# Fourteen attention pair steps reordered on five engines: conversions later, scores before transposes

## The chip, the core and the metric

The kernel runs on one core of a Trainium2 chip. The metric is device time in microseconds (us). The kernel before took 1053.33 us, the median of three runs (1053.15 to 1053.75). The program is written by hand for each engine: TensorE (PE), VectorE (DVE), ScalarE (ACT), GpSimd (POOL), and the queue of transfers on SyncE (SP). Each engine runs its instructions strictly in the order written and waits on semaphores.

## The reference

```
scores = (q @ k.T) / sqrt(64)          # 4 batches, 8 heads, 768 positions
keep   = (key < 4) | (0 <= query - key < 128)
a = softmax(where(keep, scores, -1e9));  x = (a @ v) as [3072, 512]
h = x @ w_in;  x = (h - tanh(h)) @ w_out                     # 512 -> 2048 -> 512
logits = x @ w_gate + modality_bias[modality_id]
e = argmax(logits); out = softmax(logits)[e] * (relu(x @ w1[e]) @ w2[e])   # 8 experts
```

The results must hold float32 accuracy, so operands are scaled by a power of two and split into a high and a low float16 part.

## The kernel before, in words

Attention goes by **pairs**: 128 queries of two heads. A **group** g is one head pair over 384 queries, so it has three pairs, r = 3g, 3g+1, 3g+2. The first 14 pairs (`ALONE = 14`) run before the first dense layer starts; each is a **step** r of `alone`. From pair 14 on, pairs are threaded between the matmuls of the dense layers (`window`), which fill TensorE. The first dense matmul (`mlp_in`, line 805) waits for the low part of x of group 3, which pair 11 completes; it stands behind all that PE has in the 14 steps.

What a pair needs, by function and line:

- `score_pair`: PE computes scores (L607) into one PSUM tile pair, `s_ps`. It may start only when the exponentials (L635) of the pair before have read that tile. DVE masks (L621, L625, L627) and takes the row maxima (L629). ACT takes the exponentials and row sums (L635).
- `normalise`: DVE inverts the row sums (L645, L646), ACT writes the normed rows (L652). In a step with r = 3g the normed rows also wait until DVE has copied the sink columns of the group before (`gather_sinks`, L664).
- `transpose_probs`: PE transposes (L679), ACT copies the high part (L684), DVE takes the low part (L688), POOL writes the masked copies into `pt` (L694, and L697 unless r = 3g).
- `transpose_sinks`, once a group: PE (L713), ACT (L718), DVE (L722).
- `weigh_values` (PE, L760, L762) and `split_x` (ACT L782, DVE L785).

Beside the pairs stand preparations, placed by a **half step** number i (step r holds i = 2r and 2r+1). `conversions` turns group g of q and k into halves: two maxima on DVE (L406), five small scale operations and two multiplications on POOL (L417 to L421, L432), the high halves on ACT (`conv`, L449, waits for the multiplication), the low halves on POOL (L453). `prepare_alone` does the same for v (maxima L503 on DVE, multiplication L518 on POOL, high half L533 on ACT, low half L536 on POOL), the sinks' rows of v (L542, L550, L559), and both weight matrices (L296 and L311 on PE, L358 on ACT, L361 on DVE, L365 and L367 on POOL).

A row like `ACT q_hi` that waits therefore also holds back the exponentials of the next pair, since they stand behind it on ACT.

Of the kernel before, what the change touches and what calls it, by code (L numbers as in the profile page):

```python
# [125 lines left out]
def front(nc, dram, shared, attention):  # L126

    with ExitStack() as ctx:
# [76 lines left out]
        q = {n: sem("f_" + n) for n in names}  # L205
# [338 lines left out]
        def sink_halves(E, eng, b):  # L544
            s = b % 2
            if E == "act":
                eng.wait_ge(q["vs_mult"], b + 1)
                if b >= 2:
                    eng.wait_ge(q["pv_done"], pv_count(2 * PPC * (b - 1) - 1))
                eng.activation(vs_all[s][:], vs_raw[:], ACT.Copy).then_inc(q["vs_hi_done"], 1)  # L550
            if E == "pool":
                if b == 0:
                    eng.wait_ge(q["conv_lo"], 8)
                if b:
                    eng.wait_ge(q["qk_mult"], 2 * (2 * HP * b + 1))
                    eng.wait_ge(q["parted"], parts(max(r for at, r in scored.items() if at <= SLOTS * (2 * b - 2) + 22)))
                eng.wait_ge(q["vs_hi_done"], b + 1)
                low = vs_all[s][STRIP:2 * STRIP, :]
                eng.tensor_tensor(low, vs_raw[STRIP:2 * STRIP, :], low, ALU.subtract).then_inc(q["vs_lo_done"], 1)  # L559
                eng.wait_ge(q["vs_lo_done"], b + 1)  # L560
# [18 lines left out]
        def parts(r):  # L579

            return sum(1 if is_first(i) else 2 for i in range(r + 1))

        def pv_count(r):

            return sum(not is_first(i) for i in range(r + 1))
# [601 lines left out]
        def conversions(E, eng, i):  # L1187

            for g in range(1, HP * NC):
                early = {1: (None, 0, 1, 2), 2: (4, 5, 6, 7), 3: (8, 9, 10, 11), 4: (13, 14, 15, 16), 5: (19, 20, 21, 22)}  # L1190
                q_top, k_top, q_split, k_split = early.get(g, (6 * g - 11, 6 * g - 9, 6 * g - 7, 6 * g - 6))
                tops, splits = (q_top, k_top, k_top), (q_split, k_split)
                at = divmod(g, HP)
                for part in range(2):
                    if i == tops[part]:
                        qk_top_of(E, eng, *at, part)
                if i == tops[2]:
                    qk_scales(E, eng, *at)
                    qk_multiply(E, eng, *at)
                for part in range(2):  # L1200
                    if i == splits[part]:
                        conv(E, eng, *at, part)

        def prepare_alone(E, eng, i):

            for blk in {0: (0,), 1: (1, 2), 2: (3,), 3: (4, 5)}.get(i, ()):
                v_tops(E, eng, 0, blk)
            if i == 0 and E == "pool":
                late_constants(E, eng)
            if i == (3 if E == "dve" else 4) and E in ("dve", "pe"):  # L1210
                spread(E, eng, 0)
            if i == (4 if E == "dve" else 5):
                v_scales(E, eng, 0)
                for blk in range(TPC):
                    v_multiply(E, eng, 0, blk)
            if i == 8:
                for blk in range(TPC):
                    v_split(E, eng, 0, blk)
            if i == 9:
                sink_multiply(E, eng, 0)  # L1220
            if i == 11:
                sink_halves(E, eng, 0)
            if i in (18, 20, 22):
                v_multiply(E, eng, 0, i // 2 - 6)
            if i in (19, 21, 23):
                v_split(E, eng, 0, (i - 1) // 2 - 6)
            if i in (5, 6, 7, 8):
                weight_gram(E, eng, 0, i - 5)
            if i == 10:
                weight_diagonal(E, eng, 0)  # L1230
            if i == (11 if E == "pe" else 12):
                weight_product(E, eng, 0)
            w_in_at = (13, 15, 17, 19, 21, 23, 25)
            at = i - 1 if E == "dve" else i
            if at in w_in_at:
                weight_split(E, eng, 0, w_in_at.index(at))
            if i in (12, 14, 16, 18):
                weight_gram(E, eng, 1, (i - 12) // 2)
            if i == 19:
                weight_diagonal(E, eng, 1)  # L1240
            if i == (20 if E == "pe" else 21):
                weight_product(E, eng, 1)
            if i == 22:
                batch_scales(E, eng, 0)
            if i in (23, 26):
                weight_split(E, eng, 1, (23, 26).index(i))
            if i == 26:
                if E == "dve":
                    late_constants(E, eng)
# [49 lines left out]
        def stage(work_on, E, eng, r, *more):  # L1299
            if r is not None and 0 <= r < PAIRS:  # L1300
                work_on(E, eng, r, *more)

        def alone(E, eng):

            weighed = {5: (1,), 7: (2,), 8: (4, 5)}
            if E in ("pe", "dve"):
                score_pair(E, eng, 0)
            conversions(E, eng, 0)
            for r in range(ALONE):
                if E == "pe":  # L1310
                    stage(transpose_probs, E, eng, r - 1)
                    if r + 1 < ALONE:
                        score_pair(E, eng, r + 1)
                    for of in weighed.get(r, (r - 2,) if r > 8 else ()):
                        stage(weigh_values, E, eng, of)
                if E == "act":
                    score_pair(E, eng, r)
                    stage(transpose_probs, E, eng, r - 1)
                    normalise(E, eng, r)
                if E == "dve":  # L1320
                    normalise(E, eng, r)
                    if r + 1 < ALONE:
                        score_pair(E, eng, r + 1)
                    stage(gather_sinks, E, eng, r - 1)
                    stage(transpose_probs, E, eng, r - 1)
                if E == "pool":
                    stage(transpose_probs, E, eng, r - 1)
                for i in (2 * r, 2 * r + 1):
                    if i:
                        conversions(E, eng, i)  # L1330
                    if i == 2 * r + (E in ("act", "dve")):
                        stage(transpose_sinks, E, eng, r - 1)
                    if i == 2 * r:
                        for of in weighed.get(r, (r - 2,) if r > 8 else ()):
                            stage(split_x, E, eng, of)
                    prepare_alone(E, eng, i)

        scored = {2 * (r - ALONE): r for r in range(ALONE)}

# [921 lines left out]
```

## Time and profile before

| | value |
|---|---|
| median of three runs | 1053.33 us |
| profiled execution, its own time | 1051.26 us |
| its span, first to last instruction | 1049.7 us |
| first scores to first dense matmul (14 pair steps) | 8.34 to 88.81 us |
| mean granted TensorE clock, whole span | 0.974 of full speed |
| PE busy in the span | 963.0 us, 92% |
| DVE, ACT, POOL busy | 59%, 51%, 43% |

The profiled execution is the one whose rows are shown; its span leaves 1.6 us of its time uncovered. A timeline row gives start, duration, engine, line and operation; in brackets stands how long the engine had stood idle before the row and which instruction ended that wait. Durations of neighbouring rows overlap a little, because an engine takes its next instruction before the last results have landed.

### The profile page before, as it was taken

How to read it: one execution, taken by the hardware profiler on the slowest of the kernel's cores; microseconds unless marked ns; L12 is line 12 of the kernel's file. 1: busy time of each engine (PE TensorE's matmuls, PEld its weight loads, DVE VectorE, ACT ScalarE, POOL GpSimd, SP SyncE). 2: the span in 40 equal slices, each digit the busy share in tenths (PEclk: the TensorE clock that was granted, in tenths of full speed). 3: DMA queues.
4: the chain of work that ended last, by engine and by line, in shares of the span. 5: the costliest groups of instructions: out<-in, count | busy, mean ns of one | idle time of the engine just before them, and what ended most of it. 6: DMA issues, size and time to landing. Idle time of an engine off the chain costs nothing.

```text
span 1049.7 us, 23285 instructions
## 1 busy us (share of the span) xinstructions
PE 963.0 (92%) x7646; PEld 605.3 (58%) x7646; DVE 617.0 (59%) x1573; ACT 532.2 (51%) x1329; POOL 454.1 (43%) x760
## 2 busy tenths in 40 slices
PE   3447988999999999999999999999899999899996
PEld 2333544565555565565556556555577777677773
DVE  7454876668666757776756765547584334732321
ACT  4445776656656665655665665446422223522221
POOL 5755887735535643545653631210132322222322
PEclk9776999999999999999999999999999999999998
DMA  9503121314411323322122221050215112111111
GB/s 348 190 18 108 47 62 39 101 43 129 102 47 42 90 65 108 86 67 59 42 75 58 73 60 29 2 201 21 28 35 202 51 50 55 31 50 40 50 50 39
DMA packets 50293, 78.51 MB, mean 75 GB/s; under 512 B 14688, under 2 KB 35680, under 8 KB 48672
## 3 DMA queue, kind: packets, MB, share of 16 engines
q1 hardware_dynamic: 41312, 64.01, 20.5%
q0 software_dynamic: 5728, 13.43, 4.2%
q8 instruction: 43, 0.70, 0.3%
q10 hardware_dynamic: 3168, 0.02, 0.2%
q14 instruction: 42, 0.34, 0.1%
HBM read 45.35 MB, written 14.12 MB: 57 GB/s over the span
## 4 chain that ended last, share of the span: by engine, by line
PE 69%; DVE 9%; POOL 8%; issue 6%; ACT 4%; DVEq 1%; DMA 1%; SPq 1%; ACTq 0%; POOLq 0%
PE acc L861 18%; PE h_ps L805 17%; PE h_ps L1986 5%; PE s_ps L1935 5%; PE pt_ps L1935 5%; PE acc L1986 5%; PE x_out L760 3%; PE s_ps L612 3%; PE s_ps L912 2%; PE pt_ps L679 1%; POOL pt L694 1%; POOL v_lo L536 1%; POOL v_raw L518 1%; POOL qk_raw L432 1%; PE x_out L1912 1%
## 5 line engine op out<-in xcount | busy, mean ns | idle before, releaser
L861 PE MATMUL acc<-w_out_all,g_hi 128*128 128x512 f16 x768 | 228.6, 379 | 0.0
L805 PE MATMUL h_ps<-xt_hi,w_in_all 128*128 128x384 f16 x960 | 197.2, 329 | 5.7 <-DVE g_raw L826 4.5
L861 PE MATMUL acc<-w_out_all,g_lo 128*128 128x512 f16 x384 | 146.1, 381 | 2.7 <-DVE g_lo L846 2.7
L805 PEld LDWEIGHTS h_ps<-xt_hi,w_in_all 128*128 128x128 f16 x960 | 92.7, 100 | 60.3 <-issue 3.8
L103 POOL TENSOR_TENSOR tick<-tick 1x1 f32<-1x1 f32 x83 | 16.4, 197 | 251.4 <-ACT y L2002 118.0
L861 PEld LDWEIGHTS acc<-w_out_all,g_hi 128*128 128x128 f16 x768 | 75.1, 98 | 77.8
L817 ACT ACTIVATE g_raw<-h_ps,batch_scale 128x384 f32<-128x384 f32 x120 | 69.5, 579 | 98.6 <-PE h_ps L805 98.6
L846 DVE SCALAR_TENSOR_TENSOR g_lo<-g_raw,batch_scale,g_hi 128x384 f16<-128x384 f32 x128 | 89.7, 701 | 44.6 <-ACT g_hi L836 43.4
L694 POOL TENSOR_SCALAR_AFFINE_SELECT pt<-merged 128x512 f16<-128x512 f16 x96 | 67.6, 704 | 107.3 <-DVE merged L688 107.0
L836 ACT ACTIVATE g_hi<-g_raw,batch_scale 128x384 f16<-128x384 f32 x128 | 79.0, 617 | 45.5 <-DVE g_raw L826 43.3
L805 PE MATMUL h_ps<-xt_lo,w_in_all 128*128 128x384 f16 x480 | 99.0, 330 | 0.0
L826 DVE SCALAR_TENSOR_TENSOR g_raw<-h_ps,batch_scale,g_raw 128x384 f32<-128x384 f32 x120 | 74.0, 617 | 35.6 <-ACT g_raw L817 33.6
L652 ACT ACTIVATE normed<-probs,row_sum 128x132 f32<-128x132 f32 x192 | 66.8, 395 | 29.0 <-DVE row_sum L646 20.6
L453 POOL TENSOR_TENSOR k_lo<-qk_raw,k_hi 128x524 f16<-128x524 f32 (+1 forms) x31 | 33.2, 1072 | 101.2 <-ACT k_hi L449 101.1
L684 ACT ACTIVATE merged<-pt_ps 128x256 f16<-128x256 f32 x96 | 36.6, 381 | 71.2 <-PE pt_ps L679 70.6
L635 ACT ACTIVATE probs<-s_ps,neg_max 128x132 f32<-128x132 f32 x192 | 68.6, 365 | 5.6 <-DVE neg_max L629 5.4
L805 PEld LDWEIGHTS h_ps<-xt_lo,w_in_all 128*128 128x128 f16 x480 | 47.3, 98 | 32.0 <-issue 1.4
L1899 ACT ACTIVATE xg<-xg,x_scale 128x512 f32<-128x512 f32 x23 | 16.6, 722 | 92.7 <-DVE x_undo L1896 92.7
L861 PEld LDWEIGHTS acc<-w_out_all,g_lo 128*128 128x128 f16 x384 | 37.5, 98 | 40.2 <-issue 5.2
L688 DVE TENSOR_TENSOR merged<-pt_ps,merged 128x256 f16<-128x256 f32 x96 | 39.9, 416 | 34.9 <-ACT merged L684 34.7
L627 DVE COPY_PREDICATED s_ps<-later,s_ps 128x256 f32<-128x256 int32 x80 | 34.2, 428 | 36.6 <-PE s_ps L612 30.2
L697 POOL TENSOR_SCALAR_AFFINE_SELECT pt<-merged 128x512 f16<-128x512 f16 x80 | 54.5, 681 | 0.0
(322 smaller groups left out, 2185.0 us busy)
## 6 DMA issues: line engine op xcount, KB each, us to landing
qk_raw<-in_qk SPq DMA_DIRECT2D x31, 454.0 KB, 3.5
raw<-in_w SPq DMA_DIRECT2D x16, 512.0 KB, 7.5
v_raw<-in_v SPq DMA_DIRECT2D x4, 1536.0 KB, 7.3
x_tokens<-x SPq DMA_DIRECT2D x24, 256.0 KB, 3.0
w_in_all<-in_w_in SPq DMA_DIRECT2D x4, 1024.0 KB, 10.0
w_out_all<-in_w_out SPq DMA_DIRECT2D x4, 1024.0 KB, 13.2
kh_stack<-k_hi SPq DMA_DIRECT2D x60, 65.5 KB, 2.1
kl_stack<-k_lo SPq DMA_DIRECT2D x60, 65.5 KB, 2.1
```

The costliest lines, as they stand in the source:

```text
L635: eng.activation(probs[:, r % RING, j, :], s_banks[j][:, P:KW], ACT.Exp, bias=neg_max[:, r % RING, j:j + 1], scale=1.0, accum_out=row_sum[ ...
L652: eng.activation(normed[:, 2 * t + j, :], probs[:, r % RING, j, :], ACT.Copy, scale=row_sum[:, r % RING, j, 0:1])\
L694: eng.affine_select(out=at[:, :, 1, :], in_=both, pattern=[[0, 4], [1, P]], compare_op=ALU.is_ge, fill=0.0, base=0, channel_multiplier=-1) ...
L697: eng.affine_select(out=at[:, :, 0, :], in_=both, pattern=[[0, 4], [-1, P]], compare_op=ALU.is_gt, fill=0.0, base=0, channel_multiplier=1) ...
L805: mm = eng.matmul(h_of(m, f), w16[0][:, f, x * DM + k * P:x * DM + (k + 1) * P], r[:, par, k, :], start=(i == 0), stop=(i == 3 * KD - 1))
L817: eng.activation(g_raw[:, f % 2, :], h_of(m, f), ACT.Tanh, scale=batch_scale[:, b, 0:1]).then_inc(q["tanh_done"], 1)
L826: eng.scalar_tensor_tensor(g, h_of(m, f), batch_scale[:, b, 0:1], g, ALU.mult, ALU.subtract).then_inc(q["g_done"], 1)
L836: eng.activation(g_hi[f % 2][:], g, ACT.Copy, scale=batch_scale[:, b, 1:2]).then_inc(q["g_hi_done"], 1)
L846: eng.scalar_tensor_tensor(g_lo[f % 2][:], g, batch_scale[:, b, 1:2], g_hi[f % 2][:], ALU.mult, ALU.subtract)\
L861: mm = eng.matmul(acc[t][:, :], l[f % 2][:, t * P:(t + 1) * P], w16[1][:, f, x * DM:(x + 1) * DM], start=(f == 0 and i == 0), stop=(f == N ...
L1935: mm = eng.matmul(hid_ps[c][:, (f - 4 * c) * P:(f - 4 * c + 1) * P], w[:, k, f * P:(f + 1) * P], x[p][:, k * P:(k + 1) * P], start=(i == 0 ...
L1986: mm = eng.matmul(y_ps[bank][:, :], l[:, f * P:(f + 1) * P], rhs, start=(f == 0 and i == 0), stop=(f == KF - 1 and i == 2))
```

## The change

It alters only the 14 steps of `alone` and the half step tables it reads. Nothing is computed differently, and the instruction counts of the engines stay.

- ACT: in each step `normalise(r)` now stands ahead of `transpose_probs(r - 1)`.
- PE: in each step `score_pair(r + 1)` now stands ahead of `transpose_probs(r - 1)`; the transposes of the sinks stand between the two half steps.
- ACT, DVE: `transpose_sinks` stands at the step's end; `split_x` stands behind the first half step's preparations.
- Group 2's maxima go from half steps 4, 5 to 2, 3, group 4's from 13, 14 to 14, 15. POOL's scales and multiplications of groups 2 to 5 stand one half step behind the second maximum. The conversions of ACT and POOL move from 6, 7 to 5, 6 (group 2), 10, 11 to 12, 13 (group 3), 15, 16 to 18, 19 (group 4), 21, 22 to 23, 24 (group 5).
- v's last three maxima go from half steps 2, 3 to 4, 5, its scale to 6, its multiplications to 7, its split to 9, the sinks' rows to 10 and 12. `weigh_values` of pair 1 goes from step 5 to 6.

```diff
@@ sink_halves
                 if b == 0:
-                    eng.wait_ge(q["conv_lo"], 8)
+                    eng.wait_ge(q["conv_lo"], 7)
@@ conversions
-                early = {1: (None, 0, 1, 2), 2: (4, 5, 6, 7), 3: (8, 9, 10, 11), 4: (13, 14, 15, 16), 5: (19, 20, 21, 22)}
+                early = {1: (None, 0, 1, 2), 2: (2, 3, 5, 6), 3: (8, 9, 12, 13), 4: (14, 15, 18, 19), 5: (19, 20, 23, 24)}
...
-                if i == tops[2]:
+                if i == tops[2] + (E == "pool" and 2 <= g <= 5):
                     qk_scales(E, eng, *at)
                     qk_multiply(E, eng, *at)
@@ prepare_alone
-            for blk in {0: (0,), 1: (1, 2), 2: (3,), 3: (4, 5)}.get(i, ()):
+            for blk in {0: (0,), 1: (1, 2), 4: (3,), 5: (4, 5)}.get(i, ()):
...
-            if i == 8:
+            if i == 9:
                 for blk in range(TPC):
                     v_split(E, eng, 0, blk)
@@ alone
-            weighed = {5: (1,), 7: (2,), 8: (4, 5)}
+            weighed = {6: (1,), 7: (2,), 8: (4, 5)}
...
                 if E == "pe":
-                    stage(transpose_probs, E, eng, r - 1)
                     if r + 1 < ALONE:
                         score_pair(E, eng, r + 1)
-                    for of in weighed.get(r, (r - 2,) if r > 8 else ()):
+                    stage(transpose_probs, E, eng, r - 1)
+                    for of in of_step:
                         stage(weigh_values, E, eng, of)
+                    prepare_alone(E, eng, 2 * r)
+                    stage(transpose_sinks, E, eng, r - 1)
+                    prepare_alone(E, eng, 2 * r + 1)
+                    continue
                 if E == "act":
                     score_pair(E, eng, r)
+                    normalise(E, eng, r)
                     stage(transpose_probs, E, eng, r - 1)
-                    normalise(E, eng, r)
...
-                for i in (2 * r, 2 * r + 1):
-                    if i:
-                        conversions(E, eng, i)
-                    if i == 2 * r + (E in ("act", "dve")):
-                        stage(transpose_sinks, E, eng, r - 1)
-                    if i == 2 * r:
-                        for of in weighed.get(r, (r - 2,) if r > 8 else ()):
-                            stage(split_x, E, eng, of)
-                    prepare_alone(E, eng, i)
+                if r:
+                    conversions(E, eng, 2 * r)
+                prepare_alone(E, eng, 2 * r)
+                for of in of_step:
+                    stage(split_x, E, eng, of)
+                conversions(E, eng, 2 * r + 1)
+                prepare_alone(E, eng, 2 * r + 1)
+                stage(transpose_sinks, E, eng, r - 1)
```

On ACT, from the exponentials of pair 2 to those of pair 4 (a `probs` row is a pair's exponentials, `q_hi` and `k_hi` are group 2's, `pt` the sinks' copy), before:

```order
L635 ACTIVATE probs,row_sum<-s_ps,neg_max 128x132 x2
L684 ACTIVATE merged<-pt_ps 128x256
L652 ACTIVATE normed<-probs,row_sum 128x132 x2
L635 ACTIVATE probs,row_sum<-s_ps,neg_max 128x132 x2
L684 ACTIVATE merged<-pt_ps 128x256
L652 ACTIVATE normed<-probs,row_sum 128x132 x2
L449 ACTIVATE q_hi<-qk_raw 128x384
L449 ACTIVATE k_hi<-qk_raw 128x396
L718 ACTIVATE pt<-pt_ps 128x384
```

and now:

```order
L635 ACTIVATE probs,row_sum<-s_ps,neg_max 128x132 x2
L652 ACTIVATE normed<-probs,row_sum 128x132 x2
L684 ACTIVATE merged<-pt_ps 128x256
L449 ACTIVATE q_hi<-qk_raw 128x384
L635 ACTIVATE probs,row_sum<-s_ps,neg_max 128x132 x2
L652 ACTIVATE normed<-probs,row_sum 128x132 x2
L684 ACTIVATE merged<-pt_ps 128x256
L449 ACTIVATE k_hi<-qk_raw 128x396
L718 ACTIVATE pt<-pt_ps 128x384
```

The `q_hi` of group 2 now stands ahead of pair 3's exponentials, and each `merged` stands behind the `normed` of the next pair.

On POOL, from the multiplications of group 4 (`qk_raw`) to the first v block after it, before:

```order
L432 TENSOR_SCALAR qk_raw<-qk_raw,qk_scale 128x384
L432 TENSOR_SCALAR qk_raw<-qk_raw,qk_scale 128x524
L453 TENSOR_TENSOR q_lo<-qk_raw,q_hi 128x384
L694 AFFINE_SELECT pt<-merged 128x4x128
L697 AFFINE_SELECT pt<-merged 128x4x128
L453 TENSOR_TENSOR k_lo<-qk_raw,k_hi 128x524
L694 AFFINE_SELECT pt<-merged 128x4x128
L697 AFFINE_SELECT pt<-merged 128x4x128
L518 TENSOR_SCALAR v_raw<-v_raw,v_scale 128x512
L536 TENSOR_TENSOR v_lo<-v_raw,v_hi 128x4x2x64
```

and now:

```order
L432 TENSOR_SCALAR qk_raw<-qk_raw,qk_scale 128x384
L432 TENSOR_SCALAR qk_raw<-qk_raw,qk_scale 128x524
L694 AFFINE_SELECT pt<-merged 128x4x128
L697 AFFINE_SELECT pt<-merged 128x4x128
L453 TENSOR_TENSOR q_lo<-qk_raw,q_hi 128x384
L518 TENSOR_SCALAR v_raw<-v_raw,v_scale 128x512
L453 TENSOR_TENSOR k_lo<-qk_raw,k_hi 128x524
L536 TENSOR_TENSOR v_lo<-v_raw,v_hi 128x4x2x64
```

The multiplications now lie before the two selects of pair 8, and `q_lo` lies between those selects and the multiplication of the v block.

On PE, from the scores of pair 1 on, before (the first row is the last product of pair 1's scores):

```order
L607 MATMUL s_ps<-k_hi,q_hi 128x260 x2
L679 MATMUL pt_ps<-ident,normed 128x128 x2
L607 MATMUL s_ps<-k_hi,q_lo 128x260 x2
L607 MATMUL s_ps<-k_lo,q_hi 128x260 x2
L607 MATMUL s_ps<-k_hi,q_hi 128x260 x2
```

and now:

```order
L607 MATMUL s_ps<-k_hi,q_hi 128x260 x2
L607 MATMUL s_ps<-k_hi,q_lo 128x260 x2
L607 MATMUL s_ps<-k_lo,q_hi 128x260 x2
L607 MATMUL s_ps<-k_hi,q_hi 128x260 x2
L679 MATMUL pt_ps<-ident,normed 128x128 x2
```

The transposes of a pair moved behind the scores of the pair two later.

## Rows read from the trace of the kernel before

**Rows 1.** Stretches: length, PE, PEld, DVE, ACT, POOL busy (rows), granted clock, DMA share, GB/s.
```profile
24.30:34.80 10.50, 5.72 (x74) 4.36 (x74) 5.00 (x14) 6.53 (x22) 10.31 (x16) 0.90 1.01 404
34.80:46.70 11.90, 6.76 (x52) 4.82 (x51) 6.23 (x21) 6.12 (x19) 7.53 (x13) 0.51 0.42 134
88.80:97.90 9.10, 7.59 (x28) 3.13 (x29) 2.58 (x6) 1.20 (x2) 4.58 (x9) 0.52 0.32 87
```
**Rows 2.** Who waited for whom, 8 to 89 us: total, times, longest.
```profile
PE s_ps L607 <- ACT probs L635: 25.4, 8, 5.8
ACT q_hi L449 <- POOL qk_raw L432: 11.3, 4, 4.6
```
**Rows 3.** ACT's timeline: start, duration, instruction, idle before and its releaser.
```profile
19.92 0.37 ACT L635 ACTIVATE probs<-s_ps,neg_max 128x132 f32<-128x132 f32 x1 [0.16 <-DVE neg_max L629]
...
36.13 0.52 ACT L449 ACTIVATE q_hi<-qk_raw 128x384 f16<-128x384 f32 x1 [4.64 <-POOL qk_raw L432]
...
37.84 0.35 ACT L635 ACTIVATE probs<-s_ps,neg_max 128x132 f32<-128x132 f32 x1
...
43.90 0.36 ACT L635 ACTIVATE probs<-s_ps,neg_max 128x132 f32<-128x132 f32 x1
...
62.62 0.35 ACT L635 ACTIVATE probs<-s_ps,neg_max 128x132 f32<-128x132 f32 x1
...
71.64 0.35 ACT L635 ACTIVATE probs<-s_ps,neg_max 128x132 f32<-128x132 f32 x1
...
78.26 0.63 ACT L533 ACTIVATE v_hi<-v_raw 128x512 f16<-128x512 f32 x1 [4.17 <-POOL v_raw L518]
...
85.23 0.36 ACT L635 ACTIVATE probs<-s_ps,neg_max 128x132 f32<-128x132 f32 x1
```
**Rows 4.** Timelines of ACT, PE and DVE, step 12 and the first dense matmul.
```profile
80.02 0.35 ACT L635 ACTIVATE probs<-s_ps,neg_max 128x132 f32<-128x132 f32 x1
80.96 0.40 PE L607 MATMUL s_ps<-k_hi,q_lo 64*128 64x260 f16 x2 [5.48 <-ACT probs L635]
81.83 0.43 DVE L627 COPY_PREDICATED s_ps<-later,s_ps 128x256 f32<-128x256 int32 x1 [0.62 <-PE s_ps L607]
82.65 0.20 DVE L664 COPY sinks<-normed 128x72 f32<-128x72 f32 x1
82.76 0.41 DVE L688 TENSOR_TENSOR merged<-pt_ps,merged 128x256 f16<-128x256 f32 x1
82.96 0.70 ACT L652 ACTIVATE normed<-probs,row_sum 128x132 f32<-128x132 f32 x2 [1.88 <-DVE sinks L664]
83.32 0.88 PE L713 MATMUL pt_ps<-ident,sinks 128*128 128x128 f32 x3 [0.74 <-DVE merged L688]
84.23 0.49 ACT L718 ACTIVATE pt<-pt_ps 128x384 f16<-128x384 f32 x1 [0.56 <-PE pt_ps L713]
88.81 1.46 PE L805 MATMUL h_ps<-xt_hi,w_in_all 128*128 128x384 f16 x4 [1.18 <-DVE xt_lo L785]
```
**Rows 5.** POOL's timeline: scales, multiplications, selects, low halves.
```profile
22.19 0.25 POOL L417 TENSOR_SCALAR qk_exp<-qk_top 128x2 int32<-128x2 int32 x1 [0.68 <-DVE qk_top L406]
...
23.81 1.17 POOL L432 TENSOR_SCALAR qk_raw<-qk_raw,qk_scale 128x384 f32<-128x384 f32 x2
...
26.93 0.64 POOL L694 TENSOR_SCALAR_AFFINE_SELECT pt<-merged 128x512 f16<-128x512 f16 x1
...
28.13 0.92 POOL L453 TENSOR_TENSOR q_lo<-qk_raw,q_hi 128x384 f16<-128x384 f32 x1
...
30.49 3.38 POOL L536 TENSOR_TENSOR v_lo<-v_raw,v_hi 128x512 f16<-128x512 f32 x3
...
59.09 1.08 POOL L694 TENSOR_SCALAR_AFFINE_SELECT pt<-merged 128x512 f16<-128x512 f16 x1 [2.40 <-DVE merged L688]
```
**Rows 6.** PE's timeline: the same matmuls at the higher clock.
```profile
26.99 0.29 PE L607 MATMUL s_ps<-k_hi,q_lo 64*128 64x260 f16 x2
...
100.94 0.81 PE L805 MATMUL h_ps<-xt_hi,w_in_all 128*128 128x384 f16 x4
```

More of the change, by code:

```diff
@@ L1209, in prepare_alone @@
                 late_constants(E, eng)
-            if i == (3 if E == "dve" else 4) and E in ("dve", "pe"):
+            if i == (5 if E == "dve" else 6) and E in ("dve", "pe"):
                 spread(E, eng, 0)
-            if i == (4 if E == "dve" else 5):
+            if i == (6 if E == "dve" else 7):
                 v_scales(E, eng, 0)
@@ L1215, in prepare_alone @@
                     v_multiply(E, eng, 0, blk)
-            if i == 8:
+            if i == 9:
                 for blk in range(TPC):
                     v_split(E, eng, 0, blk)
-            if i == 9:
+            if i == 10:
                 sink_multiply(E, eng, 0)
-            if i == 11:
+            if i == 12:
                 sink_halves(E, eng, 0)
@@ L1309, in alone @@
             for r in range(ALONE):
+                of_step = weighed.get(r, (r - 2,) if r > 8 else ())
                 if E == "pe":
-                    stage(transpose_probs, E, eng, r - 1)
                     if r + 1 < ALONE:
                         score_pair(E, eng, r + 1)
-                    for of in weighed.get(r, (r - 2,) if r > 8 else ()):
+                    stage(transpose_probs, E, eng, r - 1)
+                    for of in of_step:
                         stage(weigh_values, E, eng, of)
+                    prepare_alone(E, eng, 2 * r)
+                    stage(transpose_sinks, E, eng, r - 1)
+                    prepare_alone(E, eng, 2 * r + 1)
+                    continue
                 if E == "act":
                     score_pair(E, eng, r)
+                    normalise(E, eng, r)
                     stage(transpose_probs, E, eng, r - 1)
-                    normalise(E, eng, r)
                 if E == "dve":
```

## The prediction

> **What bounds the kernel now.** I read the stretches first [rows 1]. From 97.9 us on PE is full and the change touches nothing, so only the time at which the first dense matmul starts can move: 88.81 us [rows 4]. Before it no engine is full over the whole part, but POOL has 10.31 of 10.50 us busy between 24.3 and 34.8 us. Then the waits [rows 2]: PE waited 25.4 us in 8 waits for exponentials, and ACT waited 11.3 us in 4 waits to write `q_hi`, for POOL's multiplication. These are one wait seen twice. The ACT timeline shows how [rows 3]: in step 5 ACT stands 4.64 us at `q_hi` of group 3, writes the rest, and only at 37.84 takes the exponentials of pair 6, whose scores had long been masked. The same happens at 78.26 with a `v_hi` that waited 4.17 us for a multiplication of POOL. So the loop is: exponentials, next scores, mask, maxima, exponentials; and what stretches it is a conversion that stands ahead of the exponentials on ACT before POOL has made its input.
>
> Step 12 shows the loop nearly bare [rows 4]: exponentials at 80.02, scores 0.94 later, mask 0.87 later (slow clock), sinks' copy 0.82 later, normed rows 0.31 later, sinks' transposes at +3.30, their copy at +4.21, next exponentials at +5.21 (85.23) [rows 3]. A step without sinks needs about 0.94 + 0.87 + 0.82 + 0.04 = 2.7 us.
>
> **The change, step by step.** I write E(r) for the start of pair r's exponentials on ACT and carry the new orders forward by the durations of the rows.
>
> *Early, it loses.* `q_hi` of group 2 stood behind E(3); now it stands ahead. Its multiplication on POOL cannot start before the selects of pair 1, and these wait for `merged`, which on PE now stands behind scores that wait for k_lo of group 1 (18.5 us, 0.3 later than before). Transposes 0.66, high part, low part (0.41) end at 20.5; the two selects, 0.59 each net of overlap (one takes 0.64 [rows 5]), at 21.7; the five scale operations 1.62 (22.19 to 23.81) [rows 5] at 23.4; the first multiplication, half of 1.17, at 23.95. `q_hi` takes 0.43 net of overlap, so E(3) = 24.4 where it was 19.92: 4.5 us lost.
>
> *Steps with r = 3g get longer.* The normed rows wait for the sinks' copy (+2.94). The high part of the pair before used to be done by then; now it stands behind the normed rows: 0.60, then about 0.38, then the low part 0.41, a hand-over 0.15, the sinks' transposes 0.88, their copy 0.42. That is 5.8 where step 12 took 5.2. With that, and `k_hi` inside it, E(4) = 30.4. Step 4 now waits for v: multiplications of three blocks end at 33.2, the third `v_hi` ends at about 34.1: E(5) = 34.1. Against before that is still 4.6 behind.
>
> *Step 5 gives it back.* It took until 37.84 because of `q_hi`; nothing of that stands there now. The pair 6 scores are the short ones, 2.4 us: E(6) = 36.5, 1.3 ahead.
>
> *Step 6.* POOL runs the three v low halves (3.38) [rows 5] from 34.0 to 37.4, selects to 38.6, scales to 40.2, multiplications to 41.4, the sinks' rows to 42.0. ACT needs that last one: high half, `k_hi`, a weight block, the sinks' copy, together 2.0: E(7) = 44.0, where it was 43.90. The 1.3 is spent.
>
> *Steps 7 and 8* have no conversion on ACT. They end with the products for x and their high part: 4.6 and 5.3 us. E(8) = 48.6, E(9) = 53.9.
>
> *Step 9* is the new stall. In it ACT holds `v_hi` of block 3, and POOL's multiplication for it stands behind the two selects and q_lo of group 4. Normed rows at E+2.94, then 0.60, 0.38, 0.41: selects from E+4.4. The first is the long form, since DVE runs a weight's low half at once behind `merged` (1.08 against 0.64) [rows 5], so they end at E+6.1; q_lo 0.9, multiplication 0.67, `v_hi` 0.55, weight 0.61, sinks' copy 0.4: 9.2 us, E(10) = 63.1 where it was 62.62. 0.5 behind again. The Trainium skill's GPSIMD Engine Reference, section 8, Key points, says that GpSimd shares its SBUF interfaces with VectorE and contends with VectorE instructions that have two SBUF inputs; the 1.08 agrees. By that rule each select next to such a low half is long, by the shorter row none would be, and the sum would gain 0.9 over steps 9 and 11.
>
> *Steps 10 and 11* gain. Before, step 10 stood for `q_hi` of group 5 until 71.64. Now ACT waits only for a v block: low part at E+3.2, one select 0.6, multiplication 0.67, `v_hi` and a weight 1.2: 5.7, E(11) = 68.8. In step 11 two selects with the long form 1.6, multiplication 0.7, `q_hi` beside it, `v_hi` and two weight blocks 1.76 (78.26 to 80.02) [rows 3, 4]: 7.3, E(12) = 76.1 where it was 80.02. 3.9 ahead.
>
> *Steps 12 and 13.* 5.8 instead of 5.2: E(13) = 81.9. From the sinks' copy to the first dense matmul it was 88.81 - 84.23 = 4.58; nothing in it changes. The copy is at 81.5: the matmul starts at 86.1.
>
> **Sum:** 88.81 - 86.1 = 2.7 us. Balance from E(3): -4.5, steps 3 and 4 -0.1, step 5 +5.9, step 6 -1.4, steps 7 to 9 -0.4, steps 10 and 11 +4.4, steps 12 and 13 with what follows -1.2: together 2.7. The profiled execution would go from 1051.26 to 1048.6; the median of the runs stands 2.07 above it, so 1053.33 becomes 1050.6.
>
> Edits at no cost. The maxima of group 2 move into step 1, where v's maxima left: their data lands at 14.6, DVE gets there at 16.8. The load of group 4 goes out when k_lo of group 2 is done, at 31.2 instead of 29.9; ten microseconds pass before step 7 asks for it. The load of group 5 goes out at 46 instead of 40 and is asked for at step 9, 58 us. Twelve stacking transfers of group 5 follow k_lo of group 5 on SP; they land some 7 us after the first dense matmul and are read 13 us after it. If that cover of 6 were gone, pair 15's scores would hold PE.
>
> **The clock.** In the stretch 24.3 to 34.8 the granted clock is 0.90, in 34.8 to 46.7 it is 0.51, the lower of the two levels (1.2 and 2.4 GHz), after PE had stood idle in wide gaps; from 88.8 to 97.9 the dense matmuls themselves ran at 0.52 [rows 1]. A pair of score products took 0.40 at the low level and 0.29 at the high one [rows 4, 6]. I took the high level for steps 4, 5 and 9 and half of step 8. Bounds: low in all of them costs 0.35 for scores, 0.25 for transposes and 0.65 for products where they end a wait, 1.8 in all. High at the start of the dense layer gains: four matmuls take 0.81 against 1.46 [rows 4, 6], so the 20 matmuls up to 97 us save five times 0.65, 3.2. I take the levels of before there.
>
> The Trainium skill's page TensorE: Matmul & The Clock Gate, section What's actually happening, has the throttled state as the default, released by activity. With shorter gaps PE would by that rule more often be found high, which is the third rival below; the rows of before only show it low at that place.
>
> **Rivals.**
>
> *POOL backlog, slower.* Place: POOL ahead of the selects of steps 10 and 11. In my schedule POOL is free 2.5 us before step 10's low part and only 0.4 us before step 11's. If it is late there, `v_hi` waits as in step 9, and both steps take that step's 9.2: +3.5 and +1.9. The first dense matmul starts at 91.5, 2.7 later than before: 1056.0. It decides once POOL runs 3 us later than I have it. For it: POOL had 10.31 of 10.50 us filled at 24.3 to 34.8, and the early 4.5 us of idle push work back. Against: the total of POOL's work is the same, and steps 7 and 8 leave it gaps.
>
> *Gains eaten, no change.* PE stays at the low level through steps 3 to 9, so the transposes behind the scores hold ACT longer: 2.7 - 1.8 = 0.9, at 1052.4. For it: 0.51 in 34.8 to 46.7. Against: 0.90 in the stretch ahead of it.
>
> *High clock at the dense layer.* 2.7 + 3.2 gives 1047.4. For it: the part has fewer gaps. Against: PE still idles some 3 us in each of steps 9 to 12, as it did in front of 88.81.
>
> *The change only swaps stalls.* If step 9's 9.2 is too long, because the multiplication is earlier, up to 1.5 more is won; this lies in the forecast's own range.
>
> **How the numbers follow.** Forecast 0.50, own range 1049.0 to 1052.3. POOL backlog 0.14, gains eaten 0.20, high clock 0.16. A measurement of this kernel tells about 0.2% (2.1 us) from no change, so faster is below 1051.2 and slower above 1055.4. Faster: 0.38 of the forecast's 0.50 and all of the high clock, 0.54. Same: the other 0.12, the 0.20 of gains eaten, less 0.02 for its upper tail: 0.30. Slower: 0.14 and that 0.02. The range 1047.0 to 1055.6 leaves out most of the backlog and the end of the high clock, 2 in 10.
>
> **What would show it.** Right: ACT stands 3 to 4 us at `q_hi` before 24.4; the long gap before the exponentials near 36 is gone; POOL starts a v multiplication near 61 and ACT waits for it; E(12) near 76; first dense matmul near 86.1. Wrong: E(3) near 20, a gap in step 11 above 4 us at `v_hi` (backlog), score products of 0.40 throughout, or dense matmuls of 0.81 from the first on. If the part from the first dense matmul to the end is not 960.9 us within 0.5, the change reached further than I have it.

## The result, and the profile after

The changed kernel took 1049.92 us (median of 20 runs, 1047.34 to 1055.5). The kernel before, run beside it on the same chips, took 1052.88 us (20 runs, 1050.91 to 1055.87). The ratio is 0.9974 [0.9963, 0.9985]: 0.26% faster, as forecast (1050.6 against 1053.33 is also 0.26%). The single profiled execution says little of the whole: it took 1051.15 us with a span of 1049.6, which is 1.2 above its own median, while the profiled one of before was 1.6 below the median of its runs. So the two spans differ by 0.1 us, and what the change does must be read where it acts.

The same three stretches as in [rows 1], after the change:

```profile
24.30:34.80 10.50, 7.53 (x74) 5.97 (x72) 5.90 (x20) 6.71 (x23) 6.77 (x10) 1.00 0.97 387
34.80:46.70 11.90, 6.48 (x49) 4.16 (x49) 7.51 (x23) 6.03 (x21) 10.22 (x18) 0.71 0.37 121
88.80:97.90 9.10, 7.60 (x45) 3.57 (x44) 3.76 (x9) 4.35 (x12) 4.65 (x11) 0.87 0.36 93
```

POOL's full stretch has moved one stretch later: 6.77 and 10.22 us busy where it was 10.31 and 7.53. The granted clock is higher in all three; in the third a part of this comes from the dense layer having started 2.1 us before the stretch does. The waits between 8 and 87 us, beside [rows 2]:

```profile
PE s_ps L607 <- ACT probs L635: 25.6, 11, 6.0
...
ACT v_hi L533 <- POOL v_raw L518: 6.0, 3, 2.9
...
ACT q_hi L449 <- POOL qk_raw L432: 4.9, 2, 4.0
```

ACT's waits for `q_hi` fell from 11.3 to 4.9 us, of which 4.0 is the new early one. PE's wait for exponentials is as large as it was (25.6 against 25.4, in 11 waits instead of 8), and `v_hi` has three waits. ACT's timeline shows where they are, beside [rows 3]:

```profile
24.15 0.53 ACT L449 ACTIVATE q_hi<-qk_raw 128x384 f16<-128x384 f32 x1 [4.05 <-POOL qk_raw L432]
24.58 0.35 ACT L635 ACTIVATE probs<-s_ps,neg_max 128x132 f32<-128x132 f32 x1
...
34.23 0.36 ACT L635 ACTIVATE probs<-s_ps,neg_max 128x132 f32<-128x132 f32 x1
...
37.40 0.36 ACT L635 ACTIVATE probs<-s_ps,neg_max 128x132 f32<-128x132 f32 x1
...
61.56 0.63 ACT L533 ACTIVATE v_hi<-v_raw 128x512 f16<-128x512 f32 x1 [2.85 <-POOL v_raw L518]
...
63.07 0.36 ACT L635 ACTIVATE probs<-s_ps,neg_max 128x132 f32<-128x132 f32 x1
...
74.76 0.63 ACT L533 ACTIVATE v_hi<-v_raw 128x512 f16<-128x512 f32 x1 [2.50 <-POOL v_raw L518]
...
76.52 0.35 ACT L635 ACTIVATE probs<-s_ps,neg_max 128x132 f32<-128x132 f32 x1
...
82.33 0.36 ACT L635 ACTIVATE probs<-s_ps,neg_max 128x132 f32<-128x132 f32 x1
```

The stall ahead of E(3) is 4.05 us, E(6) is at 37.40 with no conversion in front of it, and in step 9 ACT stands 2.85 us at `v_hi` before E(10) at 63.07. PE's first dense matmuls, beside the last of [rows 4]:

```profile
86.66 1.46 PE L805 MATMUL h_ps<-xt_hi,w_in_all 128*128 128x384 f16 x4 [1.30 <-DVE xt_lo L785]
...
92.18 0.81 PE L805 MATMUL h_ps<-xt_hi,w_in_all 128*128 128x384 f16 x4 [1.50 <-DVE g_raw L826]
```

The dense layer starts at 86.66 (before 88.81, a lead of 2.15 us) and gets the high clock 5.5 us later, where before got it 9.1 us after its start.

### The profile page after: what moved, and what is told of

Same layout as the page of the kernel before. It is cut to its first block, busy times and chain, and to the rows that moved or that the text cites. A ratio compares the mean times of both kernels' runs of the same rounds, so it can differ in the third digit from the quotient of the medians.

```text
span 1049.6 us, 23285 instructions
## 1 busy us (share of the span) xinstructions
PE 965.3 (92%) x7646; PEld 606.5 (58%) x7646; DVE 619.6 (59%) x1573; ACT 532.5 (51%) x1329; POOL 454.9 (43%) x760
## 4 chain that ended last, share of the span: by engine, by line
PE 64%; DVE 10%; POOL 8%; issue 7%; ACT 6%; DMA 2%; DVEq 1%; ACTq 0%; POOLq 0%; SPq 0%
PE h_ps L805 17%; PE acc L861 17%; PE acc L1990 4%; PE pt_ps L1939 4%; PE h_ps L1990 4%; PE s_ps L1939 4%; PE s_ps L612 3%; PE x_out L760 3%; PE s_ps L912 2%; PE pt_ps L679 2%; ACT probs L635 1%; POOL pt L694 1%; DVE ew_lo L1635 1%; DMA slot_y<-slots 1%; POOL v_lo L536 1%
## 5 line engine op out<-in xcount | busy, mean ns | idle before, releaser
L826 DVE SCALAR_TENSOR_TENSOR g_raw<-h_ps,batch_scale,g_raw 128x384 f32<-128x384 f32 x120 | 74.0, 617 | 36.4 <-ACT g_raw L817 34.0
L635 ACT ACTIVATE probs<-s_ps,neg_max 128x132 f32<-128x132 f32 x192 | 68.8, 366 | 5.4 <-DVE neg_max L629 5.3
L627 DVE COPY_PREDICATED s_ps<-later,s_ps 128x256 f32<-128x256 int32 x80 | 34.2, 428 | 34.8 <-PE s_ps L612 30.8
```

Source lines behind the costliest of these rows:

```text
L635: eng.activation(probs[:, r % RING, j, :], s_banks[j][:, P:KW], ACT.Exp, bias=neg_max[:, r % RING, j:j + 1], scale=1.0, accum_out=row_sum[ ...
L826: eng.scalar_tensor_tensor(g, h_of(m, f), batch_scale[:, b, 0:1], g, ALU.mult, ALU.subtract).then_inc(q["g_done"], 1)
```

## The experiments

Theory: the time of the first dense matmul, below called h, is set by what stands ahead of the exponentials on ACT; the change holds a gain (the tables, which put conversions nearer to when POOL has made their input) and losses (the early `q_hi`, the longer steps with r = 3g, step 9). The rivals were POOL's load as such, and the clock. Two executions of the same changed kernel gave an h of 86.66 and 85.20 (the last runs of this section), so differences of less than 1.5 us at one h say nothing by themselves. E(r) and h come from one profiled execution of each kernel; ratios are against the kernel before in the same set of runs.

**Tables and orders apart.** The change has two halves: the tables in `conversions`, `prepare_alone` and `weighed`, and the order written in `alone`. The first kernel keeps the new tables and takes back the order:

```diff
                 if E == "act":
                     score_pair(E, eng, r)
-                    normalise(E, eng, r)
                     stage(transpose_probs, E, eng, r - 1)
+                    normalise(E, eng, r)
...
-                if r:
-                    conversions(E, eng, 2 * r)
-                prepare_alone(E, eng, 2 * r)
...
+                for i in (2 * r, 2 * r + 1):
+                    if i:
+                        conversions(E, eng, i)
+                    if i == 2 * r + (E in ("act", "dve")):
+                        stage(transpose_sinks, E, eng, r - 1)
```

> Only the half step tables are changed; the instruction orders inside a step are those of the kernel before. Theory (the prediction's): the tables carry the gain and the orders cost 0.5 to 0.6 us in each step with r = 3g. Then the first dense matmul starts near 84.5 us, earlier than the 86.66 of the changed kernel, E(3) still stands near 24.2. Rival (the orders carry the gain, since scores no longer wait behind transposes): the first dense matmul starts at 88 us or later.

It took 1043.37 us (1041.33 to 1045.19) beside 1052.14, ratio 0.9912 [0.9885, 0.9939]. Its h:

```profile
83.24 1.46 PE L805 MATMUL h_ps<-xt_hi,w_in_all 128*128 128x384 f16 x4 [1.18 <-DVE xt_lo L785]
```

That is 5.6 us ahead of before and 3.4 ahead of the whole change, 1.3 earlier than expected; E(3) at 24.07 was as expected. The second kernel keeps the new order and takes back the tables:

```diff
-                early = {1: (None, 0, 1, 2), 2: (2, 3, 5, 6), 3: (8, 9, 12, 13), 4: (14, 15, 18, 19), 5: (19, 20, 23, 24)}
+                early = {1: (None, 0, 1, 2), 2: (4, 5, 6, 7), 3: (8, 9, 10, 11), 4: (13, 14, 15, 16), 5: (19, 20, 21, 22)}
...
-            weighed = {6: (1,), 7: (2,), 8: (4, 5)}
+            weighed = {5: (1,), 7: (2,), 8: (4, 5)}
```

> Only the orders inside a step are changed; the half step tables are those of the kernel before. Theory: the stalls at q_hi of groups 3, 4 and 5 (4.6, 3.1 and 2.8 us before) stay, the steps with r = 3g are 0.6 longer, the first dense matmul starts at 90 to 91 us, and the time is 1 to 2 us above that of the kernel before. Rival (the orders carry the gain): it starts near 86.7.

It took 1056.84 us, ratio 1.005 [1.0034, 1.0066], and h came at 95.19: 6.4 us later than before. Steps 3, 6, 9 and 12 are longer than before's by 0.6, 1.5, 1.5 and 0.6, step 8 by 1.1 and the way from E(13) to h by 0.6. h is 4 to 5 us later than I expected, and the time is 4.7 us above before's instead of 1 to 2. ACT in its step 9:

```profile
62.63 0.36 ACT L684 ACTIVATE merged<-pt_ps 128x256 f16<-128x256 f32 x1
65.90 0.63 ACT L533 ACTIVATE v_hi<-v_raw 128x512 f16<-128x512 f32 x1 [2.91 <-POOL v_raw L518]
66.44 0.71 ACT L358 ACTIVATE w_in_all<-w_in_all,w_scale 128x512 f16<-128x512 f32 x1
```

The larger part of the 1.5 us in this step is the high part behind the normed rows. DVE takes the low part 3.89 us after E(9) (63.02), where in the kernel before it took it 2.76 after (58.61), and POOL's selects and the v multiplication behind them are as much later. The smaller part is the sinks' copy: the next exponentials don't read it, but on ACT they stand behind it, and it now stands at the step's end, behind the wait, where it adds 0.37 us. In step 6 it is the same: the low part, and behind it on DVE the scale of a weight for which ACT stands 1.82 us, come 1.1 to 1.2 us later, and the copy adds 0.38. The expectation had counted the late high part only for the sinks' transposes, not for what stands behind the low part on DVE and POOL. So the order costs in both settings (6.4 us at h on the old tables, 3.4 on the new), and the tables gain in both (5.6 and 8.5). The whole change is a gain of its tables from which its order takes over half: at h 3.4 of 5.6 us, in the times 0.62% of 0.88%.

**The early `q_hi`.** One entry puts group 2's high halves one half step later, behind E(3):

```diff
-                early = {1: (None, 0, 1, 2), 2: (2, 3, 5, 6), 3: (8, 9, 12, 13), 4: (14, 15, 18, 19), 5: (19, 20, 23, 24)}
+                early = {1: (None, 0, 1, 2), 2: (2, 3, 6, 7), 3: (8, 9, 12, 13), 4: (14, 15, 18, 19), 5: (19, 20, 23, 24)}
```

> The changed kernel with one entry of the table altered: group 2's conversions back to half steps 6 and 7, so that its q_hi stands behind the exponentials of pair 3. Theory (early loss is a wait of ScalarE alone): E(3) near 20.0 instead of 24.58, E(4) near 27, and 2.5 us of it are left at the first dense matmul, 84.2 instead of 86.66. Rival (GpSimd is full between 29 and 45 us and takes the lead back): E(3) near 20 but E(7) still near 45.4 and the first dense matmul within 0.5 of 86.66.

It took 1048.99 us, ratio 0.9971 [0.9958, 0.9983], the same as the whole change; h was 87.01. E(3) came at 20.10, 4.5 us earlier, but E(4) at 29.51 was only 1.0 earlier than in the changed kernel, and E(5) at 34.09 only 0.1; the expected 2.5 us at h did not come. PE shows where the first part of the 4.5 went:

```profile
18.99 0.69 PE L679 MATMUL pt_ps<-ident,normed 128*128 128x128 f32 x2
22.93 1.87 PE L296 MATMUL acc<-w_in_all 128*128 128x128 bf16 x16 [3.25 <-DVE all_top L318]
24.73 0.40 PE L607 MATMUL s_ps<-k_hi,q_lo 64*128 64x260 f16 x2
```

Pair 4's scores could have followed E(3) near 21, but a product for a weight's scale stands ahead of them and waits until 22.93 for DVE, which runs three of v's maxima from 20.48 to 22.6 first. The change itself had put them there, half steps 4 and 5 instead of 2 and 3, which the prediction did not count as a cost. That takes 3.7 us. The last 1.0 us goes at POOL, which now has both low halves of group 2 ahead of the v multiplications:

```profile
30.56 0.94 POOL L453 TENSOR_TENSOR k_lo<-qk_raw,k_hi 128x396 f16<-128x396 f32 x1
31.48 2.04 POOL L518 TENSOR_SCALAR v_raw<-v_raw,v_scale 128x512 f32<-128x512 f32 x3
```

In the changed kernel they start at 31.40, and both times E(5) stands behind the three `v_hi`. The loss at E(3), the largest single loss in the sum, is therefore worth nothing by itself: other waits lie right behind it, first PE's and DVE's, then POOL's. The rival of this run (POOL takes the lead back) had h within 0.5 of 86.66, as it came, and E(7) near 45.4, where 44.13 was measured; it holds for the last 1.0 us of the lead.

**The v multiplications one half step earlier.** In steps 9 to 11 they stood on POOL behind the two selects.

```diff
-            if i in (18, 20, 22):
-                v_multiply(E, eng, 0, i // 2 - 6)
+            if i in (17, 19, 21):
+                v_multiply(E, eng, 0, (i + 1) // 2 - 6)
```

> The changed kernel with the multiplications of v's blocks 3 to 5 one half step earlier on GpSimd (17, 19, 21), so that they stand ahead of the selects and of q_lo. Theory (steps 9, 10 and 11 stand for this multiplication): the waits of 2.85, 0.68 and 2.50 us at v_hi vanish, step 9 takes near 6.3 us instead of 9.2, steps 10 and 11 near 5, the first dense matmul starts at 82 to 83 us. Rival (GpSimd's total is the bound there): a wait of the same size appears at the sinks' copy or at q_hi, and the first dense matmul starts within 1 us of 86.66.

It took 1043.37 us, ratio 0.9919 [0.9887, 0.9951]. The three waits at `v_hi` (2.85, 0.68 and 2.50 us) are gone; step 9 took 6.2 us instead of 9.2, steps 10 and 11 5.4 and 4.7 instead of 6.3 and 7.2, and

```profile
81.50 1.46 PE L805 MATMUL h_ps<-xt_hi,w_in_all 128*128 128x384 f16 x4 [1.49 <-DVE xt_lo L785]
```

is 5.2 us ahead of the changed kernel (4.4 ahead of the mean of its two executions). The new stall of step 9 was thus real and avoidable: nothing but its place behind the selects made the multiplication late.

**Which part of the order costs.** Two kernels take back one engine's order each, on the new tables and all else of the change; each was run twice, first in one execution and then in four. ACT's (the high part ahead of the normed rows):

```diff
                 if E == "act":
                     score_pair(E, eng, r)
-                    normalise(E, eng, r)
                     stage(transpose_probs, E, eng, r - 1)
+                    normalise(E, eng, r)
```

> The changed kernel with ScalarE's order alone set back: the high part of the pair before (merged) ahead of the normed rows. Theory (the orders cost 3.4 us at the first dense matmul on the new tables, mostly because merged stands behind normed in the steps with r = 3g, where normed waits for the sinks' copy): steps 3, 6, 9 and 12 each 0.4 to 0.6 shorter, first dense matmul at 84.5 to 85.2 instead of 86.66. Rival (TensorE's order is the whole cost): it stays within 0.3 of 86.66.

> ScalarE's order alone set back, once more and timed. One look gave the first dense matmul at 84.35 us, where two looks at the changed kernel gave 86.66 and 85.20. Theory (merged behind normed is the cost of the orders, 0.3 to 0.8 in each step with r = 3g): again below 84.9, steps 6, 9 and 12 again shorter by 0.5 or more than in both looks at the changed kernel, the time near 0.993 to 0.995 of the kernel before. Rival (the look was within the 1.5 us by which the clock moves this point): 85.2 or more.

and PE's (the transposes ahead of the scores):

```diff
                 if E == "pe":
+                    stage(transpose_probs, E, eng, r - 1)
                     if r + 1 < ALONE:
                         score_pair(E, eng, r + 1)
-                    stage(transpose_probs, E, eng, r - 1)
```

> The changed kernel with TensorE's order alone set back: the transposes of a pair ahead of the next scores. Theory: ScalarE's merged no longer waits for the transposes (0.49 and 0.16 us in steps 10 and 11) and the products of steps 7, 8 and 10 come 0.4 to 0.6 earlier, first dense matmul at 85.2 to 85.9. Rival (ScalarE's order is the whole cost): within 0.3 of 86.66. A third way: scores come later behind the transposes and it is above 87.

> TensorE's order alone set back, once more and timed. One look gave the first dense matmul at 85.13. Theory (TensorE's order costs nothing that stands out of the clock's 1.5 us): between 85 and 86.7, step 12 again 5.8, the time near 0.996 of the kernel before. Rival (its order costs as much as ScalarE's): below 84.9.

With them ran the changed kernel itself once more, unaltered:

> The changed kernel once more, unaltered, to see what one more execution does. Theory (the 1.7 us lost between 165 and 190 us are the granted clock's, which fell there in one execution after an idle of 2.7 us, as it did not in the kernel before): the first dense matmul again at 86.7 within 0.1, the first dense matmul at the higher clock may come elsewhere than at 92.2, and the lead over the kernel before at 200 us lies anywhere from 1.5 to 4. Rival (the loss is one of order, a wait that the change made late): the same 1.7 us go again at the same instructions.

| kernel | h, us | step 12, us | time, us | ratio |
|---|---|---|---|---|
| changed | 86.66; again 85.20 | 5.8; 5.8 | 1049.92; one run 1047.06 | 0.9974 [0.9963, 0.9985] |
| ACT's order back | 84.35; again 83.47 | 5.1; 5.1 | one run 1044.97; 1043.55 | 0.9922 [0.9903, 0.9941] |
| PE's order back | 85.13; again 85.62 | 5.8; 5.8 | one run 1046.10; 1046.38 | 0.995 [0.9932, 0.9968] |
| tables alone | 83.24 | 5.2 | 1043.37 | 0.9912 [0.9885, 0.9939] |

The repeat of the changed kernel missed what was expected of h (86.7 within 0.1): it came 1.5 us earlier.

ACT's order alone brings back most of what the orders cost. At h, in the means of two executions, it is 2.0 of 2.7 us (85.93 for the changed kernel, 83.91 with ACT's order back, 83.24 once for the tables alone), in the times 0.52% of 0.62%. Steps 6 and 9 take 6.9 and 8.1 to 8.4 us instead of 7.5 to 8.0 and 9.2. Step 12 shows how. The changed kernel, ACT, DVE and PE, beside [rows 4]:

```profile
77.46 0.40 PE L607 MATMUL s_ps<-k_hi,q_lo 64*128 64x260 f16 x2 [6.03 <-ACT probs L635]
...
79.15 0.20 DVE L664 COPY sinks<-normed 128x72 f32<-128x72 f32 x1
...
79.47 0.70 ACT L652 ACTIVATE normed<-probs,row_sum 128x132 f32<-128x132 f32 x2 [2.15 <-DVE sinks L664]
80.07 0.36 ACT L684 ACTIVATE merged<-pt_ps 128x256 f16<-128x256 f32 x1
80.47 0.42 DVE L688 TENSOR_TENSOR merged<-pt_ps,merged 128x256 f16<-128x256 f32 x1 [1.12 <-ACT merged L684]
81.04 0.87 PE L713 MATMUL pt_ps<-ident,sinks 128*128 128x128 f32 x3 [1.34 <-DVE merged L688]
81.95 0.49 ACT L718 ACTIVATE pt<-pt_ps 128x384 f16<-128x384 f32 x1 [0.37 <-PE pt_ps L713]
```

and with ACT's order taken back, ACT and DVE:

```profile
76.66 0.38 ACT L684 ACTIVATE merged<-pt_ps 128x256 f16<-128x256 f32 x1 [1.64 <-PE pt_ps L679]
...
76.85 0.20 DVE L664 COPY sinks<-normed 128x72 f32<-128x72 f32 x1
77.07 0.42 DVE L688 TENSOR_TENSOR merged<-pt_ps,merged 128x256 f16<-128x256 f32 x1
...
77.16 0.70 ACT L652 ACTIVATE normed<-probs,row_sum 128x132 f32<-128x132 f32 x2
...
78.91 0.47 ACT L718 ACTIVATE pt<-pt_ps 128x384 f16<-128x384 f32 x1
```

In the changed kernel ACT stands 2.15 us for the sinks' copy with the ready high part queued behind it; from the sinks' copy (79.15) to the low part (80.47) is 1.32 us. With the old order ACT writes the high part inside that wait, and the low part follows the sinks' copy by 0.22 (76.85 to 77.07). PE's order moves h by 0.6 us in the mean of two, less than the 1.5 by which one kernel differs from itself: no cost of its own can be told at h. In the times the ratio with PE's order back is 0.24% lower than the change's, and the two intervals, from different sets of runs, overlap a little, so whether PE's order costs something stays open.

**The two gains together.** New tables, old order, and the multiplications early (the first and the fourth edit in one kernel):

> The new half step tables with the old orders inside a step, and v's multiplications of blocks 3 to 5 one half step earlier on GpSimd. Theory (the two gains add, since they lie in different waits): first dense matmul near 78 us (83.24 less the waits of 1.71, 0.62 and 2.87 at v_hi), the time near 0.986 to 0.990 of the kernel before. Rival (GpSimd is full by then): first dense matmul at 81 or later, no faster than either alone (0.991).

It took 1041.46 us (1038.22 to 1044.64) beside 1052.07, ratio 0.9894 [0.9876, 0.9913], the lowest ratio of all, though the intervals of the two apart reach into its own.

```profile
57.60 0.69 POOL L518 TENSOR_SCALAR v_raw<-v_raw,v_scale 128x512 f32<-128x512 f32 x1
58.25 0.64 POOL L694 TENSOR_SCALAR_AFFINE_SELECT pt<-merged 128x512 f16<-128x512 f16 x1
...
59.45 0.91 POOL L453 TENSOR_TENSOR q_lo<-qk_raw,q_hi 128x384 f16<-128x384 f32 x1
```

POOL multiplies ahead of the selects, `v_hi` waits nowhere in steps 9 to 11, and PE's wait for exponentials over the whole part is down to

```profile
PE s_ps L607 <- ACT probs L635: 9.7, 8, 2.1
```

from 25.6 us. h is at 78.87: 7.8 ahead of the changed kernel, close to the sum of the two apart (3.4 and 5.2), so at h they share little. In the time the sum shows less: against the tables alone h is 4.4 us earlier, the median 1.9.

## Why the prediction was right

| | predicted | changed kernel | again |
|---|---|---|---|
| E(3) | 24.4 | 24.58 | 24.6 |
| E(4) | 30.4 | 30.51 | 30.3 |
| E(5) | 34.1 | 34.23 | 34.1 |
| E(6) | 36.5 | 37.40 | 36.4 |
| E(7) | 44.0 | 45.39 | 43.9 |
| E(8) | 48.6 | 49.98 | 47.7 |
| E(9) | 53.9 | 53.91 | 52.1 |
| E(10) | 63.1 | 63.07 | 61.3 |
| E(11) | 68.8 | 69.36 | 67.6 |
| E(12) | 76.1 | 76.52 | 75.1 |
| E(13) | 81.9 | 82.33 | 80.9 |
| h | 86.1 | 86.66 | 85.20 |

- *Early, it loses; step 5 gives it back.* Both held within 0.2 us at E(3) to E(5). The kernel with group 2's high halves late adds what the prediction did not know: without that early loss other waits would have taken the 4.5 us by E(5) anyway, most of it one that the moved v maxima make. The prediction did not price that move, and its cost was hidden behind the early `q_hi`.
- *Steps with r = 3g, 5.8.* Step 12 took 5.81 and 5.8; with ACT's order back it took 5.1, so that order is the whole of what the step gained in length.
- *Steps 5 and 6.* E(6) was 0.9 late in one execution and right in the other: the row sums' small operation on DVE took 1.23 us (below). Step 6 was 7.5 in the sum and 8.0 and 7.5 as measured; in the longer one the sinks' copy on DVE (L664) took 0.54 us instead of 0.20.
- *Steps 7 and 8* were mis-sized: 4.6 and 5.3 in the sum, 4.6 and 3.9 measured, 3.8 and 4.4 in the other execution. In the changed kernel four products for x took 0.53 us in step 7 and 0.33 in step 8, which I had given the high level only by half. Step 8 returned the 1.4 us that steps 5 and 6 had lost, so that E(9) fitted by luck, by errors that cancel.
- *Step 9, 9.2.* Measured 9.16 and 9.2. The chain was as written. The prediction had the mechanism, not its removability:

```profile
58.29 1.09 POOL L694 TENSOR_SCALAR_AFFINE_SELECT pt<-merged 128x512 f16<-128x512 f16 x1 [1.00 <-DVE merged L688]
59.34 0.63 POOL L697 TENSOR_SCALAR_AFFINE_SELECT pt<-merged 128x512 f16<-128x512 f16 x1
59.94 0.91 POOL L453 TENSOR_TENSOR q_lo<-qk_raw,q_hi 128x384 f16<-128x384 f32 x1
60.83 0.69 POOL L518 TENSOR_SCALAR v_raw<-v_raw,v_scale 128x512 f32<-128x512 f32 x1
```

  The long select is there (1.09). In step 10 the low half of a weight starts only at 66.88, and the rows show whom it meets:

```profile
66.43 0.64 POOL L694 TENSOR_SCALAR_AFFINE_SELECT pt<-merged 128x512 f16<-128x512 f16 x1 [2.65 <-DVE merged L688]
67.05 1.13 POOL L518 TENSOR_SCALAR v_raw<-v_raw,v_scale 128x512 f32<-128x512 f32 x1
```

  The select had begun before it and took 0.64; the multiplication behind it took 1.13 where the one of step 9 took 0.69. The Trainium skill's GPSIMD Engine Reference, section 8, Key points, says that GpSimd contends with VectorE instructions of two SBUF inputs; the trace agrees with the long select and with the long multiplication.
- *Steps 10 and 11, 5.7 and 7.3.* Measured 6.3 and 7.2 (6.3 and 7.5 in the repeat): together 0.5 to 0.8 longer. The term that was too small is the multiplication of step 10: 0.67 in the sum, 1.13 in both executions. The prediction knew the long form and gave it to selects only. POOL stood idle for the low part ahead of the selects of both steps (2.65 and 0.23 us), so the rival of a POOL backlog fell.
- *Gains eaten* did not come: the lead at h was 2.15 and 3.61 us, not 0.9. The clock was higher than this rival had it: 1.00 in 24.3 to 34.8, though 0.71 in 34.8 to 46.7.
- *High clock at the dense layer* came true in half. In the changed kernel the 0.81 us matmuls began 5.5 us after h, and the lead grew from 2.15 to 3.66 us at the first product of the layer's output. In its repeat they began 9.2 us after h and the lead went from 3.61 to 3.52.
- *The part behind h* was said to be 960.9 within 0.5. It was 962.9 and 960.3. This bound was too tight rather than a sign of reach: over the ten experiments it lies between 959.0 and 963.8, with no order by lead. Here lies the 0.1 us between the two profiled spans. In the changed kernel PE fell to the low level at 164 us, and the lead fell from 3.6 to 0.7; the repeat's stayed at 3.5, so this loss is not one of order. Then before lost 1.1 us at 187.67 to a transfer (`kl_stack`) that neither execution of the changed kernel waited for, which put the repeat's lead at 4.5, outside the 1.5 to 4 that were expected. In the changed kernel's first execution, between 748 and 900 us, the expert part's waits, 1.10 us at 816.70 among them, took the rest.

The forecast of 2.7 us thus stood on a lead at h that two executions gave as 2.15 and 3.61, in the mean 2.9. That the total fits to 0.7 us is partly luck: h of one kernel moves by twice that. What carries the gain is the mechanism that was forecast, a conversion ahead of the exponentials, as the tables alone and the early multiplications show. Which entry of the tables brings how much was not run apart; by E(r) the steps that got shorter are 5, 7, 10 and 11 (8.31 to 3.17, 7.73 to 4.59, 9.02 to 6.29 and 8.38 to 7.16 us), and steps 2, 6, 9 and 12 got longer. What stays open as well: the times of some kernels gained more than h did (the tables alone 8.8 us with 5.6 at h, ACT's order back 8.3 with 5.3, the best kernel 10.6 with 9.9). One profiled execution a kernel, each up to 3 us from its median, can't say whether that is a real gain behind h.

## What to carry to other kernels

When a schedule edit has several parts, price each against the loop it sits in, and run the halves apart: here a gain of 5.6 us at h and a cost of 3.4 came as one change of 2.2. In an in-order queue, put the instruction whose input is ready ahead of the one that will wait (the high half ahead of the normed rows), and the producer ahead of the work that waits for somebody else (the multiplication ahead of the selects). Before a stall is counted as a loss, ask what waits right behind it: removing the 4.5 us at E(3) left the time the same.

## What the runs showed of the hardware

*A small VectorE instruction beside GpSimd.* In the changed kernel:

```profile
35.06 1.23 DVE L645 TENSOR_SCALAR row_sum<-row_sum 128x2 f32<-128x2 f32 x1 [0.89 <-ACT probs L635]
```

and POOL over the same time:

```profile
33.99 3.39 POOL L536 TENSOR_TENSOR v_lo<-v_raw,v_hi 128x512 f16<-128x512 f32 x3
```

In the repeat the same instruction on 128x2 elements took 0.22 us at this place:

```profile
34.91 0.22 DVE L645 TENSOR_SCALAR row_sum<-row_sum 128x2 f32<-128x2 f32 x1 [0.90 <-ACT probs L635]
```

The long one stood in the way of the normed rows and of E(6), which came 1.0 us later than in the repeat. How long the instruction takes follows a pattern. The 3.39 us are three instructions of 1.13; the second of them ends at 36.25, and the long row ends at 36.29. In the repeat the first ends at 35.08, and the short row at 35.13. From 8 to 100 us the twelve traces have 87 rows of this instruction of 0.20 us or more (up to 1.23), and every one ends within 0.06 us of the end of a GpSimd instruction; the others take 0.15 to 0.18. So where it is long, it ends with a GpSimd instruction, the running one or, as here, the next: it began 0.06 us ahead of the first one's end, in the repeat 0.17 ahead. This is read from the rows; no run moves this instruction alone.

*The clock differs between executions of one kernel.* After the same idle gap at the same place, the changed kernel and then its repeat:

```profile
163.79 0.42 PE L760 MATMUL x_out<-pt,v_hi 128*64 128x256 f16 x2 [2.69 <-POOL pt L697]
```

```profile
163.86 0.30 PE L760 MATMUL x_out<-pt,v_hi 128*64 128x256 f16 x2 [2.68 <-POOL pt L697]
```

Granted clocks from 163 to 173 us, in the same order:

```profile
163.00:173.00 10.00, 9.21 (x50) 4.69 (x51) 3.71 (x7) 3.20 (x10) 6.76 (x9) 0.66 0.01 2
```

```profile
163.00:173.00 10.00, 9.14 (x65) 5.15 (x66) 4.71 (x9) 5.22 (x13) 8.50 (x11) 1.00 0.01 2
```

With PE busy alike, 50 rows went through in one and 65 in the other. At the dense layer's start there are two outcomes as well: in the twelve traces the first 0.81 us matmul came 5.4 to 5.5 us after h in five and 9.0 to 9.2 in seven (before's among these). From h to the first product of the layer's output that is 8.5 to 8.7 us against 10.0 to 10.3, so some 1.6 us hang on it, and the changed kernel fell on either side. The Trainium skill's page TensorE: Matmul & The Clock Gate, section What's actually happening, has the low level as the default that activity lifts; these traces agree that PE is low after gaps, and show that the same gap can end either way.
